# Splitting fp32 weights in place: raw copies land where their low parts go, and first loads on three queues

## The chip, the cores and the metric

The kernel runs on one core of a Trainium2 chip. The metric is the device time of one execution in microseconds. The engines are named as in the profile: PE is TensorE (matmul), DVE is VectorE, ACT is ScalarE, POOL is GpSimd, SP is SyncE. SP, ACT and POOL can issue DMAs; "SPq" in the profile is SP issuing one.

## What is computed

Three stages in sequence, float32, 1536 tokens (batch 2 x 768) of width 512.

```python
# 1 attention, 8 heads of 64: a band of +-15 keys, and 24 block summaries (max of 32 keys, mean of 32 values)
scores_l = scale * q @ k.T, masked to abs(i - j) < 16
scores_s = scale * q @ k_sum.T + log(32)
x = softmax([scores_l, scores_s]) @ [v, v_sum]
# 2 mixture of 8 experts, top 2 by noisy logits
noisy = x @ w_gate + log1p(exp(x @ w_noise)) * noise
out[t] = sum over t's two experts e of gate[t, e] * (relu(x[t] @ w1[e]) @ w2[e])
# 3 feed-forward layer, 2048 wide
r = relu(out @ w_in);  y = (s * r * r + b) @ w_out
```

w1[e] is 512 x 1024, w2[e] 1024 x 512, w_in 512 x 2048 and w_out 2048 x 512: each expert is 4 MiB of weights, and so is each of w_in and w_out.

## The kernel before

**Three passes.** A float32 product is made as three matmuls in the type fp32r: each operand is split in a high part (what fp32r keeps) and a low part (the rest), and `three_passes` (L231 to L234) adds hi x hi, hi x lo and lo x hi. For weights the split is made like this: a piece of 128 x 1024 is loaded twice, once into a float32 buffer `raw` and once into `w_hi`, whose type keeps the high part; then `w_lo = raw - w_hi`.

**Slots and pieces.** `w_hi` and `w_lo` have two slots of 8 pieces (128 x 1024 x 4 B = 512 KB each). Expert e uses slot e % 2; w_in goes through slot 0, w_out through slot 1. `raw` (L102) has two buffers of one piece. During attention the same memory holds q and k of batch b (in w_hi's slot b) and v of batch b, `v_all[b]` (in w_lo's slot b).

**Weights on POOL.** `load_piece` (L330) issues the raw copy and the w_hi copy of piece k; `split_piece` (L340) waits for both, subtracts (L346), waits for the result and issues piece k + 2 into the raw buffer that came free. `split_weights` (L352) does eight of these for one expert, once the blocks of expert e - 2 are done. For expert 0 the split is made by DVE during attention (`split_first`, L634, called from the tile loop at L732 and after it), and POOL issues its pieces between the scatters (`next_piece`, L365):

```python
for k in {7: (0, 1), 8: (2,), 9: (3,), 10: (4,), 11: (5,)}.get(s, ()):   # DVE, tile s, L732
    split_first(k)
```

**Attention.** 12 tiles of 128 tokens, six for each batch. Per tile s: PE `scores` (L924), DVE `maxima`, ACT `exps`, PE `turn_probs` (transposes), DVE and ACT copies, PE `values` (L983), DVE `normalise` into `x_sb`, PE `turn_x` and `logits`. PE runs scores(s + 1) ahead of the rest of tile s. `means(b)` (L953) makes the block means of v and needs all of `v_all[b]`; batch 0's stands ahead of scores(0), batch 1's in tile 3. In front of means(0) stands `warm_up(72, 7)`, 72 dummy matmuls (L1028). Routing runs in groups of tiles (0 to 3, 4 to 7, 8 and 9, 10 and 11): `route_a`, `route_b`, `route_c` on DVE with `ranks` on PE give each token's two rows in `x_sorted`; POOL scatters x there, two indirect DMAs per tile (`scatter`, L358). After the last group DVE computes tables of blocks (L766 to L806).

**Order of the first loads.** All are issued by SP (L264 to L279): constants, keys of batch 0 (4 DMAs), masks, identity, v of batch 0 (3 DMAs, `load_values`, L239), queries of batch 0 (8 DMAs in two halves), gate weights, noise; then, once `rows_ready` is 1, the means are copied beside the windows of v (`spread_means`), and v, keys and queries of batch 1 follow. POOL writes zeros into the heads of `x_sorted` (8 DMAs of 256 KB, L373) after scores(2).

**Experts.** PE's loop (L1116) takes one block of 128 sorted tokens at a time, 28 blocks in this run: `up` (24 matmuls per half), transposes, `down` of the block before. DVE and ACT split x and h from PSUM. A block waits for its expert's pieces by `pieces_split`. SP loads x of the blocks and stores y.

**Feed-forward layer.** Three chunks of 512 tokens. POOL gathers each token's two expert rows (`gather`, L410), DVE mixes them; the first chunk's tiles 2 and 3 are gathered into `raw` (L413), so w_out's first pieces are loaded after DVE has read them (`mix_ready`, L426). Then POOL splits w_out. PE runs `ffn_in` for groups of four 128-wide tiles; for each of those ACT makes relu, DVE `sqr` (L890), ACT `g_hi`, DVE `g_lo` (L893); in-product i + 2 waits for relu(i). `ffn_out` of a group follows the in-products of the next group; in the first chunk it waits for w_out's pieces as well (L1172).

## Time and profile before

| | |
|---|---|
| three timed executions | 805.03, 805.19, 798.55 us; median 805.03 |
| the profiled execution | 806.26 us, span 804.60 us |
| mean granted clock of PE in the span | 0.962 of full speed |
| busy in the span | PE 752.4 us (94%), POOL 329.3 (41%), DVE 269.5 (33%), ACT 228.0 (28%) |
| moved by DMA | 131.62 MB, mean 164 GB/s |

The time of the profiled execution is the span of its trace and 1.7 us around it. A row of the timeline has the start in us from the span's start, the duration, the engine, the line of the kernel and the operation with out<-in; in square brackets stands how long the engine was idle before it and what ended that. PEclk is the granted clock of PE as a share of full speed. DMA share is the mean busy share of the core's 16 DMA engines.

### The profile page before, as it was taken

To read this page: it belongs to the slowest core of one execution; us is meant where nothing else is said; L and a number is where in the kernel's file an instruction comes from. 1 tells how busy PE (TensorE), PEld (TensorE's weight loads), DVE (VectorE), ACT (ScalarE), POOL (GpSimd) and SP (SyncE) were. 2 spreads that over 40 slices of the span, in tenths; PEclk is the share of its full clock that TensorE was granted. 3 is DMA by queue.
4 is the path that set the end of the run, shared out by engine and by line. 5 is a ranking of instruction groups with operands and counts; after the bars stand their busy time and mean duration, and the time that the engine had idled before them with its cause. 6 is when DMAs were issued, how large, how long until landed. Compare 5 with 4: busy or idle time off the path is not lost.

```text
span 804.6 us, 12449 instructions
## 1 busy us (share of the span) xinstructions
PE 752.4 (94%) x4179; PEld 590.9 (73%) x4180; DVE 269.5 (33%) x486; ACT 228.0 (28%) x493; POOL 329.3 (41%) x293
## 2 busy tenths in 40 slices
PE   8788674799999999999999999788999999999998
PEld 3366562588888888888888887476888888888886
DVE  3257676411121211212112111267441423423220
ACT  1367572122122221222212222122231422233221
POOL 0021628482764768486856767478201001000000
PEclk9798885999999999999999999889999999999999
DMA  9597637683865868587857776376212001010001
GB/s 220 124 342 248 224 119 268 216 280 80 277 196 181 275 199 280 183 264 221 274 169 251 257 255 229 117 236 186 64 39 92 14 0 53 1 52 1 1 0 53
DMA packets 52602, 131.62 MB, mean 164 GB/s; under 512 B 7470, under 2 KB 9774, under 8 KB 52570
## 3 DMA queue, kind: packets, MB, share of 16 engines
q0 software_dynamic: 32640, 98.58, 38.8%
q1 hardware_dynamic: 19930, 32.60, 13.1%
q8 instruction: 21, 0.34, 0.2%
q14 instruction: 11, 0.09, 0.0%
HBM read 109.47 MB, written 20.71 MB: 162 GB/s over the span
## 4 chain that ended last, share of the span: by engine, by line
PE 78%; DMA 8%; DVE 5%; POOL 3%; ACT 2%; issue 2%; SPq 1%; DVEq 0%; POOLq 0%; ACTq 0%
PE ps L232 23%; PE ps L234 23%; PE ps L233 23%; DMA v_all<-in_v_dram 4%; PE ps L1108 3%; DMA w_hi<-in_w_pieces_dram 2%; POOL x_sorted L362 2%; PE ps L1065 1%; DVE g_lo L893 1%; PE ps L959 1%; DVE sqr L890 1%; ACT prob L461 1%; PE ps L1132 1%; POOL w_lo L346 1%; PE ps L948 1%
## 5 line engine op out<-in xcount | busy, mean ns | idle before, releaser
L346 POOL TENSOR_TENSOR w_lo<-raw,w_hi 128x1024 fp32r<-128x1024 f32 x72 | 172.9, 2402 | 62.5 <-DMA w_hi<-in_w_pieces_dram 45.8
L232 PE MATMUL ps<-w_hi,x_hi 128*128 x224 | 91.6, 409 | 3.0 <-DVE x_lo L838 1.8
L232 PE MATMUL ps<-w_hi,h_hi 128*128 x224 | 91.0, 406 | 0.1
L846 DVE TENSOR_TENSOR h_lo<-ps,h_hi 128x1024 fp32r<-128x1024 f32 x28 | 34.3, 1225 | 169.0 <-ACT h_hi L520 169.0
L233 PE MATMUL ps<-w_lo,x_hi 128*128 x224 | 89.1, 398 | 0.0
L234 PE MATMUL ps<-w_hi,x_lo 128*128 x224 | 89.1, 398 | 0.0
L234 PE MATMUL ps<-w_hi,h_lo 128*128 x224 | 88.7, 396 | 0.0
L233 PE MATMUL ps<-w_lo,h_hi 128*128 x224 | 88.6, 395 | 0.0
L232 PE MATMUL ps<-y_hi,w_hi 128*128 128x512 f32 (+1 forms) x200 | 77.9, 390 | 4.5 <-ACT relu L543 4.4
L337 POOL DMA_DIRECT2D raw<-in_w_pieces_dram x64 | 40.8, 638 | 91.0 <-PE ps L234 33.3
L234 PE MATMUL ps<-y_hi,w_lo 128*128 128x512 f32 (+1 forms) x200 | 77.9, 389 | 0.0
L233 PE MATMUL ps<-y_lo,w_hi 128*128 128x512 f32 (+1 forms) x200 | 77.7, 388 | 0.0
L232 PE MATMUL ps<-w_hi,g_hi 128*128 128x512 f32 x192 | 76.6, 399 | 0.0
L233 PE MATMUL ps<-w_lo,g_hi 128*128 128x512 f32 x192 | 75.9, 395 | 0.0
L234 PE MATMUL ps<-w_hi,g_lo 128*128 128x512 f32 x192 | 75.9, 395 | 0.0
L890 DVE SCALAR_TENSOR_TENSOR sqr<-relu,sbb 128x512 f32<-128x512 f32 x48 | 37.8, 788 | 107.8 <-ACT relu L543 107.1
L416 POOL DMA_INDIRECT yg<-y_sorted,ypos_i x20 | 19.5, 977 | 106.8 <-DVE ymix L875 95.2
L893 DVE SCALAR_TENSOR_TENSOR g_lo<-sqr,sbb,g_hi 128x512 fp32r<-128x512 f32 x48 | 49.8, 1038 | 38.0 <-ACT g_hi L547 38.0
L511 ACT ACTIVATE ysb<-ps 128x512 f32<-128x512 f32 x28 | 16.7, 598 | 145.0 <-PE ps L234 145.0
L543 ACT ACTIVATE relu<-ps 128x512 f32<-128x512 f32 x48 | 28.6, 596 | 89.9 <-PE ps L234 89.9
L843 DVE TENSOR_SCALAR hs<-ps 128x512 f32<-128x512 f32 x28 | 19.4, 692 | 98.7 <-PE ps L234 98.7
L232 PEld LDWEIGHTS ps<-w_hi,x_hi 128*128 128x128 f32 x224 | 42.5, 190 | 12.3 <-issue 3.5
(169 smaller groups left out, 1184.4 us busy)
## 6 DMA issues: line engine op xcount, KB each, us to landing
raw<-in_w_pieces_dram POOLq DMA_DIRECT2D x64, 512.0 KB, 4.4
w_hi<-in_w_pieces_dram POOLq DMA_DIRECT2D x64, 512.0 KB, 5.1
xb<-x_sorted SPq DMA_DIRECT2D x29, 256.0 KB, 3.4
y_sorted<-ysb SPq DMA_DIRECT2D x28, 256.0 KB, 2.6
v_all<-in_v_dram SPq DMA_DIRECT2D x2, 2112.0 KB, 14.3
raw<-in_w_in_dram POOLq DMA_DIRECT2D x8, 512.0 KB, 4.8
w_hi<-in_w_in_dram POOLq DMA_DIRECT2D x8, 512.0 KB, 5.9
raw<-in_w_out_dram POOLq DMA_DIRECT2D x8, 512.0 KB, 4.5
```

The costliest lines, as they stand in the source:

```text
L232: pe.matmul(acc, l_hi, r_hi, start=start, stop=False, skip_group_check=True)
L233: pe.matmul(acc, l_hi, r_lo, start=False, stop=False, skip_group_check=True)
L234: return pe.matmul(acc, l_lo, r_hi, start=False, stop=stop, skip_group_check=True)
L337: pool.dma_start(dst, src).then_inc(raw_in[k % 2], 16)
L346: pool.tensor_tensor(w_lo[:, at:at + PIECE], raw[:, k % 2, :], w_hi[:, at:at + PIECE].bitcast(F32), ALU.subtract).then_inc(pieces_split, 1)
L416: pool.indirect_dma_start(out=dst, out_offset=None, in_=y_sorted, in_offset=bass.IndirectOffsetOnAxis(ypos_i[:, t, c:c + 1], 0)).then_inc( ...
L543: act.activation(relu[:, i % 2, :], ps[:, 4 + i % 2, :], ACT.Relu).then_inc(relu_ready, 1)
L843: dve.tensor_scalar(hs[:, 512:1024], ps[:, 2, :], 0.0, None, ALU.max).then_inc(hs_b, 1)
L846: dve.tensor_tensor(h_lo[:, :, :], ps[:, 3:5, :].rearrange("p a (k n) -> p (a k) n", n=P), h_hi[:, :, :].bitcast(F32), ALU.subtract).then_ ...
L890: dve.scalar_tensor_tensor(out=sqr[:, :], in0=relu[:, i % 2, :], scalar=sbb[:, 0:1], in1=relu[:, i % 2, :], op0=ALU.mult, op1=ALU.mult).th ...
L893: dve.scalar_tensor_tensor(out=g_lo[:, g % 2, f, :], in0=sqr[:, :], scalar=sbb[:, 1:2], in1=g_hi[:, g % 2, f, :].bitcast(F32), op0=ALU.add ...
L1108: mm = pe.transpose(ps[:, 3 + k // 4, k % 4 * P:(k % 4 + 1) * P], hs[:, k * P:(k + 1) * P], ident[:, :])
```

## The change

1. The two raw buffers go. `w_raw` is a float32 tensor at the address of `w_lo`; the raw copy of a piece lands there and is overwritten by the low part. The gathers that used `raw` get a buffer of their own, `yraw`, of the same size. Each piece has its own semaphores.
2. POOL issues all 16 transfers of an expert first (`load_weights`) and then makes the eight splits (`split_weights`) with no wait for its own result between them. The same holds for w_in and w_out; w_out's loads no longer wait for `mix_ready`.
3. Expert 0: the eight w_hi copies are issued by POOL after scores(5), ahead of all scatters; the eight raw copies by SP after values(5), since they land on v of batch 0. DVE splits one piece a tile in tiles 7 to 11 and pieces 5 and 6 after `route_c(2)`; piece 7 as before.
4. First loads: v of batch 0 is issued by ACT; keys and queries of batch 1 by POOL, once `rows_ready` is 1; the first half of batch 0's queries goes ahead of the identity on SP. The zeros for `x_sorted` move from POOL to SP, behind v of batch 1.
5. The first `warm_up` has 66 matmuls instead of 72.

```diff
-        raw = top.tensor("raw", [P, 2, PIECE], F32)
+        w_raw = nc.alloc_sbuf_tensor_at("w_raw", [P, 2 * SLOT], F32, offset=base + 2 * SLOT * 4)
+        yraw = top.tensor("yraw", [P, 2, 2 * DM], F32)
...
+        def piece(w, slot, k):
+            return w[:, slot * SLOT + k * PIECE:slot * SLOT + (k + 1) * PIECE]
...
         @block.sync
             sp.dma_start(cst[:, :], consts[:, P:]).then_inc(c_in, 16)
-            load_keys(0)
+            load_keys(sp, 0)
             sp.dma_start(msk[0:80, :], masks[0:80, :]).then_inc(m_in, 16)
+            load_queries(sp, 0, 0)
             sp.dma_start(ident[:, :], consts[:, 0:P]).then_inc(id_in, 16)
-            load_values(0)
-            load_queries(0, 0)
-            load_queries(0, 1)
+            load_queries(sp, 0, 1)
...
             spread_means(0)
-            load_values(1)
-            load_keys(1)
-            load_queries(1, 0)
-            load_queries(1, 1)
+            load_values(sp, 1)
+            sp.wait_ge(init_ready, 2)
+            for e in range(E):
+                sp.dma_start(x_sorted[e * CAP:e * CAP + P, :], zrow[:, :]).then_inc(zeros_done, 16)
             spread_means(1)
+            sp.wait_ge(pv_done, TPB)
+            for k in range(PIECES):
+                dst, rows = piece(w_raw, 0, k), w_source(0, k)
...
+                sp.dma_start(dst, rows).then_inc(raw_first[k], 16)
...
         @block.gpsimd
+            def split_piece(e, slot, k):
+                pool.wait_ge(raw_in[k], 16 * e)
+                pool.wait_ge(hi_in[k], 16 * (e + 1))
+                pool.tensor_tensor(piece(w_lo, slot, k), piece(w_raw, slot, k), piece(w_hi, slot, k).bitcast(F32), ALU.subtract).then_inc(pieces_split, 1)
+
+            def load_weights(e, slot, source):
                 for k in range(PIECES):
-                    split_piece(e, slot, source, k)
+                    load_raw(e, slot, source, k)
+                    load_hi(e, slot, source, k)
+
+            def split_weights(e, slot):
+                for k in range(PIECES):
+                    split_piece(e, slot, k)
...
-            pool.wait_ge(init_ready, 2)
+            pool.wait_ge(rows_ready, 1)
+            load_keys(pool, 1)
+            load_queries(pool, 1, 0)
+            load_queries(pool, 1, 1)
             pool.wait_ge(masks_ready, 1)
-            pool.wait_ge(scores_done, TPB // 2)
-            for e in range(E):
-                pool.dma_start(x_sorted[e * CAP:e * CAP + P, :], zrow[:, :]).then_inc(zeros_done, 16)
             pool.wait_ge(scores_done, TPB)
-            load_piece(0, 0, w_source, 0)
-            load_piece(0, 0, w_source, 1)
+            for k in range(PIECES):
+                load_hi(0, 0, w_source, k)
             pool.wait_ge(zeros_done, 16 * E)
-            scatter(0, 0, 2)
-            next_piece(2)
-            next_piece(3)
-            scatter(0, 2, 4)
-            next_piece(4)
-            next_piece(5)
-            scatter(1, 4, 6)
-            next_piece(6)
-            next_piece(7)
-            scatter(1, 6, 8)
-            scatter(2, 8, 10)
-            scatter(3, 10, 12)
+            for g in range(len(GROUP_OF)):
+                scatter(g)
             pool.wait_ge(scores_done, NT)
             pool.wait_ge(pieces_split, PIECES)
             pool.wait_ge(xb_in, 16)
-            split_weights(1, 1, w_source)
+            load_weights(1, 1, w_source)
+            split_weights(1, 1)
...
                     pool.wait_ge(pieces_split, e * PIECES)
-                    split_weights(e, slot, w_source)
+                    load_weights(e, slot, w_source)
+                    split_weights(e, slot)
...
             for t in range(TPC):
                 gather(t)
-            for k in range(2):
-                pool.wait_ge(mix_ready, 3 + k)
-                load_piece(E + 1, 1, w_out_source, k)
-            for k in range(PIECES):
-                split_piece(E + 1, 1, w_out_source, k)
+            load_weights(E + 1, 1, w_out_source)
+            split_weights(E + 1, 1)
...
         @block.scalar
+            load_values(act, 0)
             key_windows(0)
...
         @block.vector
             def split_first(k):
...
+                dve.wait_ge(raw_first[k], 16)
+                dve.wait_ge(hi_in[k], 16)
+                dve.tensor_tensor(piece(w_lo, 0, k), piece(w_raw, 0, k), piece(w_hi, 0, k).bitcast(F32), ALU.subtract).then_inc(pieces_split, 1)
...
-                for k in {7: (0, 1), 8: (2,), 9: (3,), 10: (4,), 11: (5,)}.get(s, ()):
-                    split_first(k)
+                if s >= 7:
+                    split_first(s - 7)
...
             route_c(2)
+            split_first(5)
             split_first(6)
...
         @block.tensor
-            warm_up(72, 7)
+            warm_up(66, 7)
```

## Rows read from the trace of the kernel before

**Rows 1.** The chain that ended last: shares of the span by engine.

```profile
PE 78%; DMA 8%; DVE 5%; POOL 3%; ACT 2%; issue 2%; SPq 1%; DVEq 0%; POOLq 0%; ACTq 0%
```

**Rows 2.** Busy time by stage: us, PE, PEld, DVE, ACT, POOL, PEclk, DMA share, GB/s.

```profile
66.50:147.00 80.50, 55.94 (x646) 42.01 (x647) 56.22 (x203) 44.05 (x154) 34.98 (x36) 0.77 0.59 200
...
160.00:500.00 340.00, 340.00 (x1632) 277.53 (x1630) 71.06 (x82) 76.29 (x108) 222.17 (x183) 1.00 0.72 230
...
527.00:565.00 38.00, 33.59 (x146) 26.48 (x147) 27.49 (x16) 9.77 (x16) 31.25 (x23) 0.96 0.66 198
...
565.00:804.00 239.00, 236.51 (x1040) 192.03 (x1038) 74.53 (x104) 64.66 (x100) 12.46 (x13) 1.00 0.09 30
```

**Rows 3.** Timeline, PE: start, us, instruction, idle before it and its releaser.

```profile
2.53 17.26 PE L972 MATMUL ps<-zb 128*128 128x512 bf16 x72 [2.53 <-DVE zb L590]
...
22.77 5.35 PE L959 MATMUL ps<-v_all,amean 94*32 94x512 f32 x24 [2.98 <-DMA v_all<-in_v_dram]
...
54.75 2.78 PE L959 MATMUL ps<-v_all,amean 94*32 94x512 f32 x24 [3.01 <-DMA v_all<-in_v_dram]
```

**Rows 4.** Busy time in short stretches of the loads, same columns.

```profile
3.00:6.00 3.00, 3.00 (x9) 1.09 (x8) 1.94 (x9) 0.00 (x0) 0.00 (x0) 1.00 1.00 287
...
12.00:15.00 3.00, 3.00 (x16) 1.37 (x14) 0.80 (x5) 1.39 (x4) 0.00 (x0) 1.00 1.07 215
...
41.00:44.00 3.00, 3.00 (x50) 2.65 (x47) 1.93 (x7) 2.72 (x13) 2.95 (x6) 1.00 1.04 221
...
50.00:53.00 3.00, 1.74 (x24) 1.34 (x16) 1.75 (x2) 2.10 (x6) 0.00 (x0) 1.00 1.03 409
```

**Rows 5.** Timeline, DVE: splits of expert 0's weights, and the last positions.

```profile
84.90 2.35 DVE L638 TENSOR_TENSOR w_lo<-raw,w_hi 128x1024 fp32r<-128x1024 f32 x2
...
96.28 1.23 DVE L638 TENSOR_TENSOR w_lo<-raw,w_hi 128x1024 fp32r<-128x1024 f32 x1 [5.10 <-DMA w_hi<-in_w_pieces_dram]
...
127.24 1.23 DVE L638 TENSOR_TENSOR w_lo<-raw,w_hi 128x1024 fp32r<-128x1024 f32 x1 [3.40 <-DMA w_hi<-in_w_pieces_dram]
...
135.94 0.17 DVE L716 CAST pos_i<-pos_f 128x4 int32<-128x4 f32 x1
```

**Rows 6.** Timeline, POOL: two of the issues for expert 0.

```profile
88.35 0.58 POOL L337 DMA_DIRECT2D raw<-in_w_pieces_dram  x1
...
121.59 0.77 POOL L337 DMA_DIRECT2D raw<-in_w_pieces_dram  x1
```

**Rows 7.** Timeline, PE: scores of tiles 9 and 10.

```profile
87.78 0.59 PE L943 MATMUL ps<-mskb 69*128 69x512 bf16 x2 [1.11 <-ACT prob L461]
...
88.30 1.05 PE L948 MATMUL ps<-kwin,q_sb 64*64 64x120 f32 x32
...
98.81 1.88 PE L948 MATMUL ps<-kwin,q_sb 64*64 64x120 f32 x32
```

**Rows 8.** DMA issues, 0 to 60 us: engine, op, count, KB each, median us to landing.

```profile
v_all<-in_v_dram SPq DMA_DIRECT2D x2, 2112.0 KB, 14.3
...
k_sb<-in_kT_dram SPq DMA_DIRECT2D x8, 399.0 KB, 12.1
...
cst<-in_consts_dram SPq DMA_DIRECT2D x1, 126.0 KB, 2.1
```

**Rows 9.** Timeline, POOL: expert 1's first issue, and a late expert's last split.

```profile
147.17 0.57 POOL L337 DMA_DIRECT2D raw<-in_w_pieces_dram  x1 [6.01 <-DMA xb<-x_sorted]
...
374.02 2.41 POOL L346 TENSOR_TENSOR w_lo<-raw,w_hi 128x1024 fp32r<-128x1024 f32 x1 [1.11 <-DMA w_hi<-in_w_pieces_dram]
```

**Rows 10.** Timeline: POOL, DVE and PE in the first chunk of the FFN.

```profile
532.49 3.41 DVE L893 SCALAR_TENSOR_TENSOR g_lo<-sqr,sbb,g_hi 128x512 fp32r<-128x512 f32 x1 [0.79 <-ACT g_hi L547]
...
532.89 2.45 POOL L346 TENSOR_TENSOR w_lo<-raw,w_hi 128x1024 fp32r<-128x1024 f32 x1
...
563.01 0.75 DVE L893 SCALAR_TENSOR_TENSOR g_lo<-sqr,sbb,g_hi 128x512 fp32r<-128x512 f32 x1 [0.79 <-ACT g_hi L547]
...
538.04 0.69 PE L232 MATMUL ps<-y_hi,w_hi 128*128 128x512 f32 x1 [2.00 <-ACT relu L543]
```

More of the change, by code:

```diff
@@ L208, in bass_program @@
         gd_ready, ge_ready, gates_ready = sem("gd_ready"), sem("ge_ready"), sem("gates_ready")
-        raw_in = [sem(f"raw_in{i}") for i in range(2)]
-        hi_in = [sem(f"hi_in{i}") for i in range(2)]
+        raw_in = [sem(f"raw_in{k}") for k in range(PIECES)]
+        hi_in = [sem(f"hi_in{k}") for k in range(PIECES)]
+        raw_first = [sem(f"raw_first{k}") for k in range(PIECES)]
         pieces_split = sem("pieces_split")
@@ L229, in last_block, with load_values, load_keys, load_queries @@
             return eng.value_load(t_last[0:1, 0:1], min_val=E - 1, max_val=BLOCKS - 1)
+        def load_values(eng, b):
+            windows = bass.AP(tensor=v.tensor, offset=v[b].offset, ap=[[DM, HALF + 32], [HALF * DM, HPB - 1], [1, DM]])
+            last = (HPB - 1) * HALF
+            eng.dma_start(v_all[b][0:HALF + 32, 0:HPB - 1, :], windows).then_inc(v_in[b], 16)
+            eng.dma_start(v_all[b][0:HALF, HPB - 1, :], v[b, last:last + HALF, :]).then_inc(v_in[b], 16)
+            if b == 0:
+                eng.wait_ge(init_ready, 1)
+            eng.dma_start(v_all[b][HALF:WKEYS, HPB - 1, :], v[b, S:S + 2 * PAD, :]).then_inc(v_in[b], 16)
+        def load_keys(eng, b):
+            for p in range(PAIRS):
+                eng.dma_start(k_sb[b][:, p, :], kT[b, p]).then_inc(k_in[b][p], 16)
+        def load_queries(eng, b, half):
+            at = half * S // 2
+            for p in range(PAIRS):
+                eng.dma_start(q_sb[b][:, p, at:at + S // 2], qT[b, p, :, at:at + S // 2]).then_inc(q_in[b][half], 16)
+        def w_source(e, k):
+            rows = w_pieces[bass.ds(e * PIECES + k, 1), :]
+            if k < KD:
+                return rows.rearrange("o (p n) -> p (o n)", p=P)
+            return rows.rearrange("o (k p n) -> p (o k) n", p=P, n=DM)
+        def w_in_source(e, k):
+            return w_in[k // 2 * P:(k // 2 + 1) * P, k % 2 * PIECE:(k % 2 + 1) * PIECE]
+        def w_out_source(e, k):
+            return w_out[k * 2 * P:(k + 1) * 2 * P, :].rearrange("(k p) n -> p k n", p=P)
+        def piece(w, slot, k):
+            return w[:, slot * SLOT + k * PIECE:slot * SLOT + (k + 1) * PIECE]
         def three_passes(pe, acc, l_hi, l_lo, r_hi, r_lo, start, stop):
@@ L316, in _ @@
         def _(pool):
-            def w_source(e, k):
-                piece = w_pieces[bass.ds(e * PIECES + k, 1), :]
-                if k < KD:
-                    return piece.rearrange("o (p n) -> p (o n)", p=P)
-                return piece.rearrange("o (k p n) -> p (o k) n", p=P, n=DM)
-            def w_in_source(e, k):
-                return w_in[k // 2 * P:(k // 2 + 1) * P, k % 2 * PIECE:(k % 2 + 1) * PIECE]
-            def w_out_source(e, k):
-                return w_out[k * 2 * P:(k + 1) * 2 * P, :].rearrange("(k p) n -> p k n", p=P)
@@ new lines, in load_hi @@
+            def load_hi(e, slot, source, k):
+                dst, src = piece(w_hi, slot, k), source(e, k)
+                if len(src.shape) == 3:
+                    dst = dst.rearrange("p (k n) -> p k n", n=DM)
+                pool.dma_start(dst, src).then_inc(hi_in[k], 16)
+            def split_piece(e, slot, k):
+                pool.wait_ge(raw_in[k], 16 * e)
+                pool.wait_ge(hi_in[k], 16 * (e + 1))
+                pool.tensor_tensor(piece(w_lo, slot, k), piece(w_raw, slot, k), piece(w_hi, slot, k).bitcast(F32), ALU.subtract).then_inc(pieces_split, 1)
@@ L359, in scatter @@
+            def load_weights(e, slot, source):
+                for k in range(PIECES):
+                    load_raw(e, slot, source, k)
[3 more added lines that the diff above has]
+                    split_piece(e, slot, k)
+            def scatter(g):
                 pool.wait_ge(pos_ready, g + 1)
-                for t in range(at, to):
+                for t in range(*GROUP_OF[g]):
                     for c in range(2):
@@ L412, in gather @@
                     if 2 <= t < TPC:
-                        dst, come = raw[:, t - 2, c * DM:(c + 1) * DM], yraw_in[t - 2]
+                        dst, come = yraw[:, t - 2, c * DM:(c + 1) * DM], yraw_in[t - 2]
                     else:
@@ L861, in mix_tile @@
                     dve.wait_ge(yraw_in[k - 2], 32)
-                    first, second = raw[:, k - 2, 0:DM], raw[:, k - 2, DM:2 * DM]
+                    first, second = yraw[:, k - 2, 0:DM], yraw[:, k - 2, DM:2 * DM]
                 else:
```

53 lines of the change are left out of this document (8 added, 45 removed).

## The prediction

> **What bounds the kernel now.** I read the chain of waits first: 78% of it is PE, 8% DMA, 5% DVE, 3% POOL [rows 1]. So PE sets the time, but something like a fifth is waits. The busy time by stage says where [rows 2]: from 160 to 500 us, the expert blocks, PE is busy 340.00 of 340.00 us, and from 565 us on 236.51 of 239. Nothing done to weights or queues can help there; it can only hurt. What can be won lies in three places:
> - 0 to 66.5 us, where PE waits for v twice (2.98 and 3.01 us of idle, ended by the DMA) [rows 3];
> - 66.5 to 147 us, where PE is busy 55.94 of 80.50 us at a mean granted clock of 0.77 [rows 2];
> - 527 to 565 us, PE 33.59 of 38 us [rows 2].
>
> All sums are against the profiled execution, 806.26 us (span 804.60); it is 1.2 us above the median of the three runs, 805.03.
>
> **Part 1: expert 0's weights during attention.** This is the largest term. DVE splits these pieces between its attention steps. Its timeline shows idle time that ends in the landing of w_hi three times: 5.10, 3.40 and, at 131.48, 1.77 us [rows 5] (two of the three rows stand there). The cause is on POOL [rows 6]: with two raw buffers a piece is issued only after an earlier split, and POOL issues it between scatters, so the pair for piece 2 goes out at 88.35 and pieces 4 onward follow their splits. After the change all eight w_hi copies go out when scores(5) is done (about 61 us) and all eight raw copies when values(5) is done (about 75 us, because they land where v of batch 0 stands), the latter from SP. Eight raw pieces are 4.19 MB: at the 409 GB/s of 50 to 53 us that is 10.3 us, at the 215 of 12 to 15 us 19.5 us [rows 4], so piece k is there at 77 + 1.3k to 77 + 2.4k us. DVE wants piece 0 at 84.9 [rows 5] and then one per tile, 6 or more us apart. Covered by 5 us at least. Step by step:
> - The 5.10 us in tile 8 goes whole: DVE is the engine that everything behind it waits for. -5.1.
> - Tile 7 splits one piece instead of two (2.35 us for two [rows 5]); PE idled 1.11 us there before scores(9) [rows 7]. -1.0.
> - After the 5.10 us PE ran at the low clock: the same 32 score matmuls took 1.88 us instead of 1.05 [rows 7]. DVE has its routing chain beside it, so I count only part of the lost PE time: -1.5 (bounds 0, and -2.7, the excess of the chain's PE pieces between 103.7 and 112 us at this ratio).
> - Behind the loop: pieces 5 and 6 are split back to back, 2 x 1.13 us, instead of after a wait of 3.40 us; piece 7 without its 1.77 us. pos_ready of the last group moves from 136.1 to about 132.9. POOL, which has 16 scatters from group 1 on at 1.27 us each, must keep up: it no longer issues four weight copies among them (0.77 us each, 3.0 us [rows 6]), so its first twelve end at about 133.1 and the last four can start behind pos_ready at 133.2, as now they start behind it at 136.4. Both limits move alike: -3.2.
>
> Sum of part 1: -10.8. Bounds: the DMA idle alone, with the tail capped by POOL if its scatters don't close up, -6.9; everything with the full clock effect, -12.
>
> **Part 2: the first loads.** v of batch 0 is issued at about 1 us by ACT instead of at 4.87 by SP behind keys; ACT has nothing to do until the keys are there, so its three issues are hidden. Means(0) on PE starts when v is there, 22.77 now [rows 3]. But the engines that move the data are already full: DMA share 1.00 at 3 to 6 us and 1.07 at 12 to 15 us [rows 4], so a second issuer starts v earlier and takes the time from the keys. What must have landed before v completes: v, keys, mask and constants, 4302 KB or 4.41 MB, and with an equal share up to all of the first half of the queries, 5.19 MB [rows 8] (the mask is 280 KB, v's two smaller parts 188 KB and a query load 192 KB by their shapes). At 287 GB/s (keys alone, 3 to 6 us) the smaller is 15.4 us, at 215 (v alone, 12 to 15 us) the larger is 24.1 us [rows 4]; with about 2.2 us before bytes flow (the constants' landing [rows 8]) v is there at 17.6 to 26.3. I take the middle: 4.8 MB at 250 GB/s is 19.2, so 21.5 us, and -1.2. Keys land later than now but ahead of v, and their sums on DVE are hidden by it. The bounds: warm_up with 66 matmuls ends at 2.53 + 17.26 x 66/72 = 18.35, so no better than -4.4; if the clock is then still high, the 24 matmuls of the means take 2.78 instead of 5.35 us as they do for batch 1 [rows 3], and the next PE steps about 1.7 less: -8.7. The other end is 26.3: +3.5.
>
> The Trainium skill, "DMA: Bandwidth & Descriptors", section "Issuing engines are not separate DMA queues", speaks against this part: transfers started by several engines run on the same 16 DMA engines and interleave, so only issue time is saved. By that rule alone part 2 would be worth about nothing, 0 instead of -1.2; the full DMA share in [rows 4] agrees with it.
>
> **Part 3: batch 1's loads.** v(1) is still issued by SP behind rows_ready and the spreading of the means; it lands at 54.7 and PE waits 3.01 us for it [rows 3]. New: keys and queries of batch 1 are issued by POOL at the same moment, not behind v, and the zeros move from POOL to SP, behind v. Until v lands, v and the means' copies (2.85 MB) and the part of keys and queries that shares with them must move; with 2.7 MB of that at 280 GB/s, between the 221 and the 409 GB/s of [rows 4], it takes 19.8 us from 35 us: 54.8. I take 0. Low end: v keeps the engines for itself, 2.85 MB at 221 GB/s (41 to 44 us [rows 4]) is 12.9 us, PE's wait goes: -3.0, and the DVE's sums of keys are late next. High end: all 6.06 MB at 221 is 27.4 us, v at 62.4: +7.7. SP's wait for values(5) sits ahead of the y zeros alone; they are needed at block 3. POOL's twelve issues (0.56 us each) stand ahead of nothing due before 61 us.
>
> **Part 4: experts 1 to 7 and w_in.** Now POOL alternates issue, wait and split; an expert takes 35 to 41 us (the one whose loads start at 335.0 has its last split at 374.02 to 376.4 [rows 9]). New: 16 issues, at 0.56 to 0.77 us each 9 to 12 us, then eight splits of 2.40 us, 19.2 us: some 31 us, the first four done after about 21. PE spends 12.5 us a block, at least three blocks an expert, 37.5 us, and has no wait now [rows 2]. Cost 0, gain 0. The one tight place is expert 1, whose loads start at 147.17 [rows 9]: first w1 half at 168, needed at 184.7. If the issues were held back until the data had drained (8.4 MB at 261 GB/s, 32 us) the first half would come at 147 + 32 + 9.6 = 189: +4; I give that little weight. DVE's steps here read PSUM and are not slowed by POOL's splits.
>
> **Part 5: w_out beside the first chunk of the FFN.** Here POOL hurts DVE. sqr and g_lo read two SBUF tiles; g_lo takes 0.75 us alone but 3.41 at 532.49, ending 0.56 us after POOL's split of 532.89 [rows 10]. The tile then takes 4.15 us instead of about 2.75, and PE waits 2.00 us for relu there and 1.02 and 1.12 us two and three tiles on [rows 10] (the first of them). All eight splits fall on tiles already. New: issues from 520.3, 16 x 0.75 = 12 us, then splits from 532.3 without POOL's issue gap of 1.75 us, one every 2.5 to 3.2. sqr and g_lo of one tile then fall into two different splits: (2.45 + 0.56) x 2 = 6.0 us a tile instead of 4.15, but tiles 0 and half of 1 go free. Followed through, relu(5), which frees PE's last in-product, comes at 552.4 instead of 550.5: +1.8. Bounds: -2.0 if sqr follows g_lo within one gap (4.05 us a tile), +9.9 if POOL keeps the port through eight splits (8 x 2.45 = 19.6 us without DVE, relu(5) at 560.4).
>
> The Trainium skill, "SBUF — State Buffer", section "Who interferes with whom", says that a DVE operation with two SBUF inputs and a GpSimd operation that reads SBUF hold the shared pair one at a time, whole instructions, and that issue order decides. The 3.41 us row agrees. It does not say who wins when POOL has its next split ready, which is the difference between +1.8 and +9.9.
>
> **Sum.** -10.8 - 1.2 + 0 + 0 + 1.8 = -10.2: 796.1 against the profiled 806.26, and 794.8 against the median. Own range, from the bounds of the parts taken as independent: 787 to 802.
>
> **Rivals.**
> - The first loads do overlap well: v at 18.4 with a warm PE (-8.7), and v(1) without a wait (-3.0). 806.3 - 10.8 - 11.7 + 1.8 - 1.2 = 784.4. For: 409 GB/s at 50 to 53 us, with two queues of different work, against 215 [rows 4]. Against: the DMA share is already full.
> - POOL keeps the port in part 5: +9.9 instead of +1.8, 802.9. For: g_lo started 0.4 us before the split and still waited for it. Against: until now DVE came through after every split.
> - Slower: keys and queries take engine time from v in both batches at v's own slow rate. v(0) at 26.3 (+3.5), v(1) at 62.4 (+7.7), and with over 10 us of PE idle ahead of it the low clock costs 1 or 2 us more. 806.3 - 10.8 + 3.5 + 7.7 + 1.8 + 1.5 - 1.2 = 808.8. It decides once the two v's are together more than 9 us late. For: v alone already runs at 215 with a full share. Against: in the mix at 50 us 409 was reached.
> - The loads of expert 0 are late after all (raw pieces behind values(5)): part 1 falls to about -3, 802.6. It would show as DVE idle before w_lo.
>
> **How the numbers follow.** Forecast 0.46, overlap 0.27, port kept 0.13, slower 0.09, late loads 0.05. About 1% (8 us) is what a measurement of this kernel can tell from no change. Under 797.0 lie most of the forecast (0.30) and the overlap case; over 813.1 only the slower case with further losses. Faster 0.58, same 0.37, slower 0.05. The range: 783 to 806 leaves out the slower case and the far end of the overlap.
>
> **What would show it.** Right: no DVE idle before w_lo in 80 to 135 us, the last scatter near 131 instead of 141, PE at 1.05 us for its score matmuls in tiles 9 and 10; v(0) landing between 18 and 26; PE 340 of 340 in the blocks; splits of w_out from about 532, g_lo at 3 us for a few tiles. Wrong: v(1) later than 58 us; any PE idle before up or down in the blocks; g_lo over 5 us.

## The result and the profile after

The changed kernel takes 819.51 us (median of 4 runs, 818.99 to 820.67), the kernel before 805.11 in the runs beside it: ratio 1.0197, 95% interval 1.014 to 1.0254. It is slower, by 1.4 to 2.5%, where 794.8 us, range 783 to 806, was predicted. The profiled execution took 818.99 us, its span is 817.1 us, 12.5 us over the 804.60 of before. The parts of the change lie in different stretches of the span and can be read there.

The chain that ended last, changed kernel; it answers to [rows 1]. PE has a larger share, DMA 6 instead of 8%, POOL 1 instead of 3%:

```profile
PE 82%; DMA 6%; DVE 6%; ACT 2%; issue 2%; POOL 1%; SPq 1%; POOLq 0%; ACTq 0%; DVEq 0%
```

Busy time by stage, changed kernel, same stretches and columns as [rows 2]:

```profile
66.50:147.00 80.50, 59.59 (x707) 44.90 (x707) 61.26 (x210) 45.96 (x157) 35.32 (x40) 0.84 0.68 227
160.00:500.00 340.00, 339.85 (x1630) 277.15 (x1629) 70.48 (x82) 76.26 (x108) 212.98 (x174) 1.00 0.65 222
527.00:565.00 38.00, 19.60 (x80) 15.72 (x79) 29.64 (x13) 8.42 (x14) 24.90 (x15) 0.73 0.57 178
565.00:804.00 239.00, 239.00 (x1051) 194.30 (x1050) 76.78 (x107) 64.00 (x99) 11.47 (x12) 1.00 0.07 23
```

The expert blocks are full as before. The tail of attention is better: clock 0.84 instead of 0.77. The stretch 527 to 565 us is where it goes wrong: PE 19.60 us of work instead of 33.59.

PE's timeline, changed kernel; the first two rows answer to the two means of [rows 3]:

```profile
20.11 2.78 PE L953 MATMUL ps<-v_all,amean 94*32 94x512 f32 x24 [1.71 <-DMA v_all<-in_v_dram]
...
54.23 5.35 PE L953 MATMUL ps<-v_all,amean 94*32 94x512 f32 x24 [9.54 <-DMA v_all<-in_v_dram]
...
64.20 1.88 PE L942 MATMUL ps<-kwin,q_sb 64*64 64x120 f32 x32
...
72.30 1.05 PE L942 MATMUL ps<-kwin,q_sb 64*64 64x120 f32 x32
...
549.37 0.79 PE L268 MATMUL ps<-y_hi,w_hi 128*128 128x512 f32 x1 [18.40 <-ACT relu L538]
```

v of batch 0 comes early and finds PE at full clock: the means take 2.78 us instead of 5.35. v of batch 1 comes at the old time, but PE has waited 9.54 us for it and runs at the lower level afterwards: 5.35 us for the means, 1.88 for the scores at 64.20. The last row is the large loss, a wait of 18.40 us for relu. The granted clock during the wait for v(1), in stretches of 3 us:

```profile
48.00:51.00 3.00, 0.00 (x0) 0.00 (x0) 0.00 (x0) 0.00 (x0) 0.00 (x0) 0.81 1.05 212
51.00:54.00 3.00, 0.00 (x0) 0.00 (x0) 0.00 (x0) 0.00 (x0) 0.00 (x0) 0.50 1.06 340
```

It falls from 2.4 to 1.2 GHz (0.50) while PE, and every other engine, waits.

Four points in time split the 12.5 us. The second and third are the first and the last turn of a block, which one row gives for each kernel (instruction, count, durations, first and last start), before and then after:

```profile
L1065 PE MATMUL ps<-ident,xb x116: 270/272/305, 146.7 to 491.0; 128*128 128x128 f32 x116
```

```profile
L1059 PE MATMUL ps<-ident,xb x116: 270/272/302, 142.4 to 488.2; 128*128 128x128 f32 x116
```

| stretch | before, us | after, us | difference | forecast |
|---|---|---|---|---|
| start to scores(6) | 66.99 | 72.30 | +5.3 | -1.2 (parts 2, 3) |
| scores(6) to first block | 79.7 | 70.1 | -9.6 | -10.8 (part 1) |
| first to last block | 344.3 | 345.8 | +1.5 | 0 (part 4) |
| last block to the end | 313.6 | 328.9 | +15.3 | +1.8 (part 5) |

Each column is one profile. Two profiles of one program, e5 and e11 below, differ by 3.9 us in the first stretch and by 2.5 in the second, so the first two differences are good to a few microseconds only.

DVE in the first chunk of the FFN, changed kernel, and then POOL beside it; they answer to [rows 10]:

```profile
527.46 20.62 DVE L884 SCALAR_TENSOR_TENSOR sqr<-relu,sbb 128x512 f32<-128x512 f32 x1 [2.53 <-ACT relu L538]
548.87 0.75 DVE L887 SCALAR_TENSOR_TENSOR g_lo<-sqr,sbb,g_hi 128x512 fp32r<-128x512 f32 x1 [0.79 <-ACT g_hi L542]
```

```profile
528.89 18.63 POOL L355 TENSOR_TENSOR w_lo<-w_raw,w_hi 128x1024 fp32r<-128x1024 f32 x8
```

One `sqr` that needs 0.75 us takes 20.62. It ends at 548.08, 0.56 us after the last of POOL's eight splits at 547.52. In [rows 10] a g_lo ended 0.56 us after one split in the same way. There some 1.75 us lay between two splits: POOL's wait for its own result (0.30) and two issues. Now the splits follow each other directly, and DVE waits for all eight.

### The profile page after: what moved, and what is told of

It reads as the page before. It is cut to its first block, busy times and chain, and to the rows that moved or that the text cites. A ratio compares the mean times of both kernels' runs of the same rounds, so it can differ in the third digit from the quotient of the medians.

```text
span 817.1 us, 12416 instructions
## 1 busy us (share of the span) xinstructions
PE 751.1 (92%) x4173; PEld 592.8 (73%) x4174; DVE 273.4 (33%) x486; ACT 228.7 (28%) x493; POOL 322.0 (39%) x289
## 3 DMA queue, kind: packets, MB, share of 16 engines
q1 hardware_dynamic: 19821, 33.33, 12.8%
## 4 chain that ended last, share of the span: by engine, by line
PE 82%; DMA 6%; DVE 6%; ACT 2%; issue 2%; POOL 1%; SPq 1%; POOLq 0%; ACTq 0%; DVEq 0%
PE ps L268 24%; PE ps L270 24%; PE ps L269 24%; DMA v_all<-in_v_dram 5%; PE ps L1102 3%; DVE sqr L884 3%; PE ps L1059 2%; PE ps L1007 1%; PE ps L953 1%; PE ps L1126 1%; ACT prob L455 1%; PE ps L999 1%; PE ps L942 1%; PE ps L974 1%; PE ps L990 1%
## 5 line engine op out<-in xcount | busy, mean ns | idle before, releaser
L355 POOL TENSOR_TENSOR w_lo<-w_raw,w_hi 128x1024 fp32r<-128x1024 f32 x72 | 170.7, 2468 | 5.3 <-DMA w_hi<-in_w_pieces_dram 3.4
L268 PE MATMUL ps<-y_hi,w_hi 128*128 128x512 f32 (+1 forms) x200 | 78.7, 393 | 18.4 <-ACT relu L538 18.4
L884 DVE SCALAR_TENSOR_TENSOR sqr<-relu,sbb 128x512 f32<-128x512 f32 x48 | 56.0, 1166 | 117.8 <-ACT relu L538 117.6
L840 DVE TENSOR_TENSOR h_lo<-ps,h_hi 128x1024 fp32r<-128x1024 f32 x28 | 34.3, 1225 | 169.0 <-ACT h_hi L515 169.0
L344 POOL DMA_DIRECT2D w_raw<-in_w_pieces_dram x56 | 36.9, 659 | 105.7 <-PE ps L270 98.2
L268 PEld LDWEIGHTS ps<-y_hi,w_hi 128*128 128x128 f32 x200 | 39.1, 195 | 26.7 <-ACT relu L538 18.8
L350 POOL DMA_DIRECT2D w_hi<-in_w_pieces_dram x64 | 42.2, 665 | 33.4 <-PE ps L942 32.9
```

Source lines behind the costliest of these rows:

```text
L268: pe.matmul(acc, l_hi, r_hi, start=start, stop=False, skip_group_check=True)
L344: pool.dma_start(dst, src).then_inc(raw_in[k], 16)
L350: pool.dma_start(dst, src).then_inc(hi_in[k], 16)
L355: pool.tensor_tensor(piece(w_lo, slot, k), piece(w_raw, slot, k), piece(w_hi, slot, k).bitcast(F32), ALU.subtract).then_inc(pieces_split, 1)
L840: dve.tensor_tensor(h_lo[:, :, :], ps[:, 3:5, :].rearrange("p a (k n) -> p (a k) n", n=P), h_hi[:, :, :].bitcast(F32), ALU.subtract).then_ ...
L884: dve.scalar_tensor_tensor(out=sqr[:, :], in0=relu[:, i % 2, :], scalar=sbb[:, 0:1], in1=relu[:, i % 2, :], op0=ALU.mult, op1=ALU.mult).th ...
```

## The experiments

Times are medians; "ratio" is against runs of the kernel before on the same chip. A difference between kernels that ran on different chips is given by medians and by ratios where the two differ. They stand in the order of what they settle.

**e1: a gap between w_out's splits.** POOL waits for its own result before each next split, as it did before the change.

```diff
-            split_weights(E + 1, 1)
+            for k in range(PIECES):
+                if k:
+                    pool.wait_ge(pieces_split, (E + 1) * PIECES + k)
+                split_piece(E + 1, 1, k)
```

> In the changed kernel sqr of the first tile stood from 527.5 to 548.1 us beside w_out's eight splits. Theory A (POOL's splits follow each other so closely that the shared SBUF port never comes free for DVE): a wait of POOL for its own result between two splits opens a gap of about 0.3 us, in which DVE gets the port. Then no sqr or g_lo takes over 4 us, tiles take 4 to 6 us while the splits run, and the total falls by 8 to 15 us, to 805 to 811 us. Theory B (POOL holds the port for as long as its queue has such work, gaps of 0.3 us make no difference): sqr still takes about 20 us and the total stays at 819 us.

Measured: 810.12 us, ratio 1.0029 [0.9997, 1.0062]; 9.4 us less than the changed kernel by the medians, 1.7% by the ratios. POOL, and then DVE, in e1:

```profile
525.89 22.09 POOL L355 TENSOR_TENSOR w_lo<-w_raw,w_hi 128x1024 fp32r<-128x1024 f32 x8
```

```profile
529.15 2.71 DVE L887 SCALAR_TENSOR_TENSOR sqr<-relu,sbb 128x512 f32<-128x512 f32 x1
532.64 1.98 DVE L890 SCALAR_TENSOR_TENSOR g_lo<-sqr,sbb,g_hi 128x512 fp32r<-128x512 f32 x1 [0.79 <-ACT g_hi L545]
534.73 2.70 DVE L887 SCALAR_TENSOR_TENSOR sqr<-relu,sbb 128x512 f32<-128x512 f32 x1
```

Eight splits take 22.09 us instead of 18.63. From the start of one to the start of the next it is 2.77 us instead of 2.30, 0.47 more. A record of a split lasts 2.52 us (median) in the changed kernel, longer than the step, so the records overlap; in e1 it lasts 2.70, and they don't. That is the "gap" of this document: it is not seen as idle time, and how much of the 0.47 us is POOL's wait and how much DVE's turn isn't shown. It is enough: DVE gets one operation through per split, each waiting for one split only. PE waits for relu 8.1 us in four pieces instead of 18.4 in one.

**e2: the same, without POOL's reads.** The low parts of w_out are set to zero by memset; they are not computed.

```diff
-            split_weights(E + 1, 1)
+            for k in range(PIECES):
+                pool.wait_ge(raw_in[k], 16 * (E + 1))
+                pool.wait_ge(hi_in[k], 16 * (E + 2))
+                pool.memset(piece(w_lo, 1, k).bitcast(F32), 0.0).then_inc(pieces_split, 1)
```

> This run leaves the splits of w_out out: POOL writes zeros into the low parts instead (eight memsets, no SBUF input), at the same place and after the same loads. Theory A (what blocks DVE's sqr is POOL reading SBUF through the shared port): no sqr or g_lo of the first tiles takes over 1 us, PE has no wait of over 1 us for relu, total 798 to 804 us. Rival (any burst of POOL instructions, or POOL's issues of transfers, holds DVE): sqr takes at least as long as the memsets, some 8 us, and some of the 18.4 us of PE idle stays.

Measured: 799.44 us (one run). POOL and then DVE in e2:

```profile
531.54 3.08 POOL L426 MEMSET w_lo<- 128x1024 f32 x3
```

```profile
529.31 0.75 DVE L887 SCALAR_TENSOR_TENSOR sqr<-relu,sbb 128x512 f32<-128x512 f32 x1 [2.47 <-ACT relu L541]
530.86 0.75 DVE L890 SCALAR_TENSOR_TENSOR g_lo<-sqr,sbb,g_hi 128x512 fp32r<-128x512 f32 x1 [0.79 <-ACT g_hi L545]
531.72 0.75 DVE L887 SCALAR_TENSOR_TENSOR sqr<-relu,sbb 128x512 f32<-128x512 f32 x1
```

Three memsets back to back leave sqr at 0.75 us, and no wait of PE for relu is left. So it isn't POOL's writing, nor the 16 transfers that land at the time.

**e8: one source instead of two.** Each split is a copy of the raw piece; the low parts are not computed.

```diff
-            split_weights(E + 1, 1)
+            for k in range(PIECES):
+                pool.wait_ge(raw_in[k], 16 * (E + 1))
+                pool.wait_ge(hi_in[k], 16 * (E + 2))
+                pool.tensor_copy(piece(w_lo, 1, k), piece(w_raw, 1, k)).then_inc(pieces_split, 1)
```

> The changed kernel with each of w_out's eight splits replaced by a copy of the raw piece, one source in SBUF in place of two (the low parts are then not computed). Theory A (any GpSimd operation that reads SBUF back to back holds VectorE off): sqr still takes as long as the copies last, near 8 copies, and the run stays above 810 us. Theory B (only operations with two sources do): sqr and g_lo take 0.75 us as in e2, no wait for relu, 799 to 801 us.

Measured: 801.41 us (one run). POOL and then DVE in e8:

```profile
531.00 3.33 POOL L426 CAST w_lo<-w_raw 128x1024 fp32r<-128x1024 f32 x3
535.53 1.10 POOL L426 CAST w_lo<-w_raw 128x1024 fp32r<-128x1024 f32 x1 [1.21 <-DMA w_hi<-in_w_out_dram]
```

```profile
531.81 3.07 DVE L890 SCALAR_TENSOR_TENSOR g_lo<-sqr,sbb,g_hi 128x512 fp32r<-128x512 f32 x1 [0.79 <-ACT g_hi L545]
534.98 0.75 DVE L887 SCALAR_TENSOR_TENSOR sqr<-relu,sbb 128x512 f32<-128x512 f32 x1
```

The total looks like theory B, but the rows speak for A: while three copies follow each other, g_lo takes 3.07 us and ends 0.55 us after the third (531.00 + 3.33). e2's three memsets, just as close and nearly as long (3.08 us), left g_lo and sqr at 0.75 us. The later copies wait for w_hi 1.2 to 1.7 us each, so they have gaps: g_lo then takes at most 1.06 us. That is why the total, which theory A put above 810 us, came out low; a copy lasts 1.04 to 1.11 us where a split takes 2.3. Reading SBUF without a gap is the condition; one source will do.

**e3: keys and queries of batch 1 behind v(1) on SP.** POOL's issues of them go; the zeros follow them.

```diff
             load_values(sp, 1)
+            load_keys(sp, 1)
+            load_queries(sp, 1, 0)
+            load_queries(sp, 1, 1)
             sp.wait_ge(init_ready, 2)
...
-            load_keys(pool, 1)
-            load_queries(pool, 1, 0)
-            load_queries(pool, 1, 1)
```

> Keys and queries of batch 1 are issued by SP behind v of batch 1 again, the zeros behind them. Theory A (v of batch 1 is late because keys and queries now share the DMA engines with it): v lands about 13 to 16 us after its issue instead of 23.3, PE's 9.5 us of idle before the means of batch 1 falls to 0 to 3 us and the means take 2.8 us instead of 5.35; total lower by 6 to 12 us. Theory B (v is late because of its own slow rate or of the copies of the means ahead of it): v lands 20 us or more after its issue as now, and the total stays within 2 us; keys being later could cost up to 5 us.

Measured: 801.98 us, ratio 0.9948 [0.9916, 0.998]; 17.5 us less than the changed kernel by the medians, 2.5% by the ratios, more than the 6 to 12 us expected. v(1) lands 14.1 to 14.7 us after its issue instead of 23.3 to 23.6. PE's timeline in e3:

```profile
45.86 2.78 PE L953 MATMUL ps<-v_all,amean 94*32 94x512 f32 x24
...
58.11 1.05 PE L942 MATMUL ps<-kwin,q_sb 64*64 64x120 f32 x32
```

The means start 8.4 us earlier and without a wait. They and what follows run at the full clock, so scores(6) starts at 58.11 instead of 72.30: 14.2 us, of which 8.4 are the landing and 5.8 the clock. The first block starts at 128.7 instead of 142.4. DVE's stall in the FFN is untouched (21.21 us).

**e7: keys and queries on POOL, but after v(1).** This tells the sharing of the DMA engines from the second queue itself.

```diff
             pool.wait_ge(rows_ready, 1)
+            pool.wait_ge(v_in[1], 48)
             load_keys(pool, 1)
```

> The changed kernel with POOL's keys and queries of batch 1 held until v(1) has landed; they stay on POOL's queue. Theory (they cost v(1) their share of the engines, as they fly at the same time): v(1) lands 13 to 15 us after its issue, means(1) has no idle time before it or under 1 us, the run is 802 to 806 us. Rival (it is the second queue itself, or the zeros behind v(1) on SP): v(1) still takes over 20 us and the run stays at 818 to 821 us. If the keys now come too late, ScalarE waits for them at tile 6 and the summaries of batch 1 stall VectorE in tiles 3 and 4: 808 to 815 us.

Measured: 808.31 us, ratio 1.0048 [1.0016, 1.008]. PE's timeline in e7:

```profile
45.86 2.78 PE L954 MATMUL ps<-v_all,amean 94*32 94x512 f32 x24 [0.51 <-DMA v_all<-in_v_dram]
```

v(1) takes 13.4 to 14.8 us though the zeros still follow it on SP and POOL's queue is still used. It is the flying at the same time that costs. Now the keys are late, as the expectation's last case says: DVE waits 6.5 us for them before a sum and ACT 3.6 before its windows, and PE, idle for 3.86 us ahead of the next scores, goes on at the lower clock (1.88 us at 55.52). So scores(6) starts at 64.07 us, 6.0 later than in e3. Between the whole runs e7 and e3 lie 6.3 us by the medians, 1.0% (8 us) by the ratios. SP's queue, v first and keys straight behind, does both.

**e4: v(0) back on SP behind the keys.** The first half of the queries is behind v(0) again and the warm-up has 72 matmuls, the rest is as in the changed kernel.

```diff
+            sp.dma_start(ident[:, :], consts[:, 0:P]).then_inc(id_in, 16)
+            load_values(sp, 0)
             load_queries(sp, 0, 0)
-            sp.dma_start(ident[:, :], consts[:, 0:P]).then_inc(id_in, 16)
...
-            load_values(act, 0)
...
-            warm_up(66, 7)
+            warm_up(72, 7)
```

> v of batch 0 is issued by SP behind the identity again, queries behind it, 72 warm-up matmuls. Theory A (the second issuing queue made v land at 20.1 instead of 22.8, and with the clock still high it saved the slow means): means(0) starts at 22.5 to 23 and takes 5.35 us, scores(1) is 7 us later than in the changed kernel; but v of batch 1 is then waited for as long as before the shift (9.5 us of idle), so the total rises by 5 to 8 us. Rival B (the page's rule that issuing from several engines saves only issue time, v lands early for another reason): means(0) starts within 1 us of 20.1.

Measured: 824.4 us, ratio 1.0204 [1.015, 1.0259], which overlaps the changed kernel's: 4.9 us more by the medians, 0.1% by the ratios, where 5 to 8 us were expected. PE's timeline in e4:

```profile
23.27 5.35 PE L953 MATMUL ps<-v_all,amean 94*32 94x512 f32 x24 [3.72 <-DMA v_all<-in_v_dram]
...
61.46 5.35 PE L953 MATMUL ps<-v_all,amean 94*32 94x512 f32 x24 [9.51 <-DMA v_all<-in_v_dram]
```

The means of batch 0 start 3.2 us later and take 5.35 us again. The wait for v(1) is 9.51 us as before: v(1) is issued 7 us later and lands 7 us later, so it has no other cause in the first loads. How much of this reaches the end stays inside the error here; e9 asks again where the clock and the FFN are in order.

**e5: e3 and the splits of w_out placed.** Pieces 0 and 1 with a gap, 2 to 5 behind DVE's work on in-products 0 to 7, 6 and 7 behind that on 8 to 11. There PE has `ffn_out` to do and DVE nothing.

```diff
-            split_weights(E + 1, 1)
+            for k in range(PIECES):
+                if k == 1:
+                    pool.wait_ge(pieces_split, (E + 1) * PIECES + 1)
+                if k == 2:
+                    pool.wait_ge(glo_ready, 2 * FG)
+                if k == 6:
+                    for t in (TPC, TPC + 1):
+                        pool.wait_ge(mix_ready, t - 1)
+                        gather(t)
+                    pool.wait_ge(glo_ready, 3 * FG)
                 split_piece(E + 1, 1, k)
-            for t in range(TPC, NT):
+            for t in range(TPC + 2, NT):
```

> Keys and queries of batch 1 on SP behind v(1) (as in e3), and w_out's splits put where VectorE has nothing to do: pieces 0 and 1 with a gap between them, pieces 2 to 5 once glo_ready is 8, 6 and 7 once it is 12. Theory (the back-to-back splits hold VectorE off, nothing else is wrong in the FFN): sqr in the first chunk falls from 21.2 us to at most 3 us, TensorE's wait of 19.0 us for relu to under 3 us and the cold clock behind it goes; e2 without the reads was 20 us under the changed kernel, so this comes to 802 - (20 - 2) = 784 us, 782 to 788. Rival (PE then waits for w_out's low parts instead, as the splits come later): a wait of some 5 to 10 us ahead of the first products with w_out, 789 to 795 us.

Measured: 788.3 us, ratio 0.98 [0.9757, 0.9844], 0.3 us above the 782 to 788 of the theory; e3 is 13.7 us higher by the medians, 1.5% by the ratios. POOL and then DVE in e5:

```profile
516.69 5.43 POOL L358 TENSOR_TENSOR w_lo<-w_raw,w_hi 128x1024 fp32r<-128x1024 f32 x2
539.87 9.43 POOL L358 TENSOR_TENSOR w_lo<-w_raw,w_hi 128x1024 fp32r<-128x1024 f32 x4 [17.76 <-DVE g_lo L897]
...
562.27 5.38 POOL L358 TENSOR_TENSOR w_lo<-w_raw,w_hi 128x1024 fp32r<-128x1024 f32 x2 [7.66 <-DVE g_lo L897]
```

```profile
519.97 2.69 DVE L894 SCALAR_TENSOR_TENSOR sqr<-relu,sbb 128x512 f32<-128x512 f32 x1
523.45 0.75 DVE L897 SCALAR_TENSOR_TENSOR g_lo<-sqr,sbb,g_hi 128x512 fp32r<-128x512 f32 x1 [0.79 <-ACT g_hi L552]
...
537.50 0.75 DVE L894 SCALAR_TENSOR_TENSOR sqr<-relu,sbb 128x512 f32<-128x512 f32 x1 [0.46 <-ACT relu L548]
...
551.49 0.75 DVE L894 SCALAR_TENSOR_TENSOR sqr<-relu,sbb 128x512 f32<-128x512 f32 x1 [11.70 <-ACT relu L548]
```

Four splits back to back fall into the 11.70 us in which DVE has nothing, and no one waits for them. PE waits 2.3 us for relu once and never for a low part. This beats both kernels, by 2% the one before.

**e11, e10 and e9: a twin, the gap alone, v(0) on SP.** e11 is e5 again, on the chip of the other two. e10 is e3 with e1's edit and no gate. e9 is e5 with e4's edit.

> e5_gated once more, to compare with the two beside it on one chip. Both theories: 786 to 791 us, 2.0% under the kernel before.

> e3 with POOL waiting for its own result between w_out's splits (e1's edit), and nothing put later. Theory: e3's 802 us less the 9.4 us that the same edit gave in e1, 791 to 795 us; so the gate of e5 is worth some 4 to 5 us beyond the gap. Rival (the gap does all of it, the gate nothing): within 2 us of e11.

> e5_gated with v(0) back on SP behind the keys. Theory (v(0) on ScalarE's queue is a gain that reaches the end: in e4 it took 3 us from means(0) and 7 us from the first rows): 4 to 7 us over e11, 791 to 797 us. Rival (the tail behind attention takes it back, what is left is what a median of 805 us can't show): within 2 us of e11.

| run | us | ratio | interval | scores(6) | first block |
|---|---|---|---|---|---|
| e5 | 788.3 | 0.98 | 0.9757 to 0.9844 | 57.68 | 130.7 |
| e11 | 789.41 | 0.982 | 0.9771 to 0.987 | 61.61 | 137.1 |
| e10 | 795.09 | 0.9925 | 0.9892 to 0.9958 | 59.61 | 130.4 |
| e9 | 793.17 | 0.9896 | 0.9864 to 0.9929 | 63.98 | 135.1 |

The gate is worth 5.7 us over the gap alone: the intervals don't meet. What the gap alone is worth on top of e3 the totals don't settle: e10 is 6.9 us under e3 by the medians, but only 0.2% by the ratios, and these intervals overlap. In its profile PE waits 9.1 us for relu in five pieces, where in e3 it waits 19.0 in one. v(0) on ACT (with the order of the queries and the warm-up that belong to it) is worth 3.8 us against e11 and 4.9 against e5 by the medians; its interval and e11's just touch, so "about 4, not well measured". The twins e5 and e11 differ by 6.4 us at the first block in their profiles and by 1.1 in their medians: one profile doesn't measure a few microseconds of attention.

**e6 and e12: part 1 undone.** Both start from e5. In e6 only expert 0's high parts go out in pairs between the scatters, the raw copies stay on SP. In e12 both are issued by POOL in pairs, and DVE splits them at the tiles of the kernel before.

```diff
-            for k in range(PIECES):
-                load_hi(0, 0, w_source, k)
+            pool.wait_ge(pv_done, TPB)
+            load_first(0)
+            load_first(1)
             pool.wait_ge(zeros_done, 16 * E)
-            for g in range(len(GROUP_OF)):
-                scatter(g)
+            scatter(0, 0, 2)
+            next_piece(2)
+            next_piece(3)
+            scatter(0, 2, 4)
...
-                if s >= 7:
-                    split_first(s - 7)
+                for k in {7: (0, 1), 8: (2,), 9: (3,), 10: (4,), 11: (5,)}.get(s, ()):
+                    split_first(k)
```

> e5_gated with expert 0's high parts issued two at a time between the scatters again, each pair after the split two before; the raw copies stay early. Theory (part 1 of the prediction: issuing them all at once is worth 5.1 us of waits, and with the clock and the tail up to 10.8 us): VectorE waits again before splits in the last tiles, and the block loop starts 4 to 9 us later than in e5_gated, so does the end. Rival (the scatters and the tables bound the tail whatever the weights do): the first block starts within 2 us of e5_gated's.

> e5_gated with the whole of part 1 undone: expert 0's raw and high copies issued by POOL two pieces at a time between the scatters, the first pair behind values(5), and the splits on VectorE at the tiles where the kernel before has them. Theory (part 1 is worth what the traces show from scores(6) to the first block, 79.7 us before against 70 to 75.5 us in the kernels with it): that stretch is 77 to 82 us again with waits of several us before w_lo, and the run is 5 to 9 us over e5_gated's 788.3 to 789.4, 794 to 798 us. Rival (what e6 left open: the stretch is set by the clock and the routing chain, which vary by 5 us between twins, and the weights' issue matters little): within 3 us of e5_gated, no wait before w_lo over 2 us.

Measured: e6 791.47 us, ratio 0.9838 [0.9798, 0.9878], 3.2 us over e5 and 2.1 over e11 where 4 to 9 were expected, and inconclusive: it overlaps both, and its first block at 135.8 us lies between the twins'. DVE waited only 0.46 and 1.20 us before w_lo. e12 795.71 us, ratio 0.989 [0.985, 0.993]: 7.4 us over e5 and 6.3 over e11 by the medians, 7.2 and 5.6 by the ratios. The interval lies above e5's and overlaps e11's by 0.002. From scores(6) (57.44) to the first block (139.5) it takes 82.1 us, where 79.7 were seen before and 70.1 in the changed kernel. DVE's timeline in e12:

```profile
120.60 1.26 DVE L658 TENSOR_TENSOR w_lo<-w_raw,w_hi 128x1024 fp32r<-128x1024 f32 x1 [1.64 <-DMA w_hi<-in_w_pieces_dram]
...
124.31 1.22 DVE L658 TENSOR_TENSOR w_lo<-w_raw,w_hi 128x1024 fp32r<-128x1024 f32 x1 [0.79 <-DMA w_hi<-in_w_pieces_dram]
```

The size is part 1's, but the waits before w_lo come to 2.4 us only, not to the several that the theory named. Three scores, at 66.02, 83.09 and 92.83 us, took 1.88 us as at the lower clock; in e5 two did. Which part of the 6 to 7 us is the waits and which the clock behind them stays open; that part 1 as a whole gains about that much is shown against e5, and against e11 only just not beyond the error.

## Why the prediction was wrong

**Part 5, +1.8, measured +15.3: the step that failed.** I took it that DVE gets through after every split, as in [rows 10], and gave "POOL keeps the port" a bound of +9.9 and a chance of 0.13 as a rival. The change took away both things that lay between two splits, POOL's wait for itself and the two issues; e1 shows that the wait alone, 0.47 us from start to start, keeps DVE going. e2 and e8 show that POOL's reads are the cause. My argument against the rival, "until now DVE came through after every split", was drawn from a kernel that had the gap. It named a row and not its condition. The bound was also too small: I let tiles 0 and 1 go free, with splits from 532.3 us. They began at 528.89, and even the very first sqr did not end before they did, so PE had the fewest in-products in hand, and it waited 18.40 us where the four waits of before sum to 4.4. That is +14.0. Behind the wait twelve matmuls took 0.63 us or more instead of 0.39, as at the lower clock, where before eight did behind the wait of 2.00 us: about 1 us more. The bound had DVE's time about right (19.6 us without it, measured 20.62) and PE's loss too small.

The Trainium skill, "SBUF — State Buffer", section "Who interferes with whom", lets a DVE operation with two SBUF inputs contend with a GpSimd operation that reads SBUF and not with one that only writes; e2's 0.75 us beside memsets agrees. It says that issue order decides. Here an sqr that by the profile had started 1.4 us before the first split lost to all eight (spans on POOL are rough), and in e1, e5, e10 and e11 one that had started 1.1 to 2.2 us before the first split got through 0.31 to 0.33 us after that split's start. So issue order alone doesn't tell the outcome.

**Part 3, 0, and part 2, -1.2; together measured +5.3.** v(1) landed at 54.2 us; I had 54.8. That agreement is luck: I let the loads start at 35 us and take 19.8; they started 7 us earlier, at 27.9, and took 26.3, near my upper bound of 27.4. In that time 7.0 MB moved, at 267 GB/s, where I had let 5.55 MB (v, the copies and 2.7 MB beside them) move at 280. And only the time of landing was forecast, which was the wrong quantity. Part 2 did better than forecast: v(0) landed at 20.1 us (I took 21.5 between 17.6 and 26.3) and found a warm PE, the 2.78 us of the "overlap" rival. So the tiles of batch 0 ran some 7 us earlier, and PE's wait for a v(1) at the old time grew from 3.01 to 9.54 us. After that PE was at the lower level: from the means to scores(6) 18.1 us instead of 12.2. I had given a clock loss to the slower rival alone, where v(1) comes late, and had put it at 1 or 2 us; e3 shows 5.8. It goes with the wait and not with the time of landing. The length of the wait alone doesn't fix it either: behind 2.98 us ahead of means(0) PE was at the lower level and behind 3.01 us ahead of means(1) it wasn't [rows 3]. The share of the engines was right in kind: keys and queries lengthened v(1)'s flight from 15.8 us to 23.6, and e3 and e7 each took that back, to 14.7 and 14.8 at most.

Why v(0) came early: the same 3 us stretches as in [rows 4], changed kernel.

```profile
12.00:15.00 3.00, 3.00 (x16) 1.35 (x15) 0.95 (x1) 0.00 (x0) 0.00 (x0) 1.00 1.05 296
15.00:18.00 3.00, 3.00 (x15) 1.37 (x14) 0.95 (x1) 0.00 (x0) 0.00 (x0) 1.00 1.07 273
```

At the same full DMA share 296 GB/s are moved where v, with the keys landed, had 215. A busy share of 1.0 is no measure of what the engines can carry. That v's packets go through faster when they are mixed with keys and queries fits these rows, and the 212 GB/s of 48 to 51 us, when the keys and most queries of batch 1 had landed (medians 7.6 and 12.8 us after their issue, which ended at 33.8); no run isolates it. The Trainium skill, "DMA: Bandwidth & Descriptors", section "Issuing engines are not separate DMA queues", leaves only issue time to be saved. The run doesn't speak against it: v's first issue came at 0.92 us instead of 4.87, 4.0 us earlier, and v(0) was there 2.7 us earlier. My reading of the rule, that it leaves about nothing, left this issue time out.

**Part 1, -10.8, measured -9.6** in that stretch of the trace, and 5.6 to 7.4 us at the end of the run by e12. The mechanism held: no DVE idle before w_lo. The clock and the tail may have been counted somewhat high; a second profile of the same kernel can differ by several microseconds.

**Part 4, 0, measured +1.5** from the first block to the last. It lies in the second block: the first ran at a mean clock of 0.86 in both kernels, but in the 5 us behind it (155 to 160 us) the clock was 0.66 instead of 1.00 and PE started 13 matmuls instead of 20. From 160 us on PE was busy without a gap. Why the clock fell there once more is open. The splits in a row cost nothing there: DVE's h_lo, which reads PSUM and one tile of SBUF, took 1225 ns before and after.

**The whole.** The losses of parts 5 (13.5 us over forecast), 2 and 3 (6.5), 4 (1.5) and 1 (1.2) are the 22.7 us between -10.2 and +12.5. Two rivals, "POOL keeps the port" and the slower one, each had one of the mechanisms, the latter without the right size, and I treated them as alternatives; they sit in different stages, so both could come true, and did. Such terms should be added in the range.

## What to carry to other kernels

When a change removes a wait of an engine for itself, ask who lived in that gap: here GpSimd splits in a row that read SBUF held VectorE's operations on two SBUF tiles until the last of them. A wait of GpSimd for its own result, 0.47 us from start to start, let one through per split; a gate that puts the splits where VectorE is idle ended it. Issue from one queue, in order of need, what must land in order of need; here a second queue gained about 4 us for v(0) (e9) and cost 17.5 us for v(1), where keys and queries took engine time from the transfer that PE was waiting for (e3). A wait of TensorE that grew from 3 to 9.5 us cost itself and 5.8 us of clock behind it, so forecast the wait and not the landing.

## What was unexpected of the hardware

- VectorE can be held off through eight GpSimd operations in a row (20.62 us for an operation of 0.75), and through three copies with one source (3.07 us, e8). Memsets do not hold it.
- That sqr started 1.4 us before the first split, while POOL still issued transfers, and did not end before it. In e2 the same operation took 0.75 us beside such issues; with the gap between the splits (e1, e5, e11) it took 1.39 to 1.64 us and was through 0.31 to 0.33 us into the first of them. Why it didn't get through here, and in e3 (21.21 us), is open.
- With keys and queries beside v 296 and 273 GB/s were moved, where v with the keys landed had 215, at the same busy share.
